# Rounded and remaining parts of w_out side by side: weight loads of the outputs step by two elements

## The reference

```python
qn = q / (np.linalg.norm(q, axis=1, keepdims=True) + 1e-06)
kn = k / (np.linalg.norm(k, axis=1, keepdims=True) + 1e-06)
s = kn.transpose(0, 2, 1) @ qn / tau          # B x 256 x 256
a = softmax(s, axis=-1)                        # written out in the reference
x = (v @ a).reshape(12032, 256)
h = x @ w_in                                   # 256 -> 2048
g = h * (1.0 / (1.0 + np.exp(-h)))
out = g @ w_out                                # 2048 -> 256
```

## Time and profile before

| | |
|---|---|
| median of 3 runs | 1107.22 us |
| profiled execution, its own time | 1106.86 us |
| its span (first to last instruction) | 1105.1 us |
| PE (matmuls) busy | 1096.5 us, 99% |
| PEld (weight loads) busy | 1080.7 us, 98% |
| DVE, ACT, POOL busy | 739.7, 646.0, 32.3 us |
| weight loads of the outputs | 3072, 188 ns each in the record |

### The profile page before, as it was taken

The page is one execution under the profiler, slowest core; times in us unless marked ns, Lnnn a source line. Parts: engine busy times, 40 slices in busy tenths (PEclk is TensorE's granted clock), DMA queues, the critical chain, the costliest instruction groups (busy, mean ns, idle before and its releaser), DMA issues.

```text
span 1105.1 us, 16789 instructions
## 1 busy us (share of the span) xinstructions
PE 1096.5 (99%) x6252; PEld 1080.7 (98%) x6252; DVE 739.7 (67%) x1188; ACT 646.0 (58%) x973; POOL 32.3 (3%) x24
## 2 busy tenths in 40 slices
PE   8999999999999999999999999999999999999998
PEld 7888999999999999999999999999999999999998
DVE  5776796666666665666687786666666666666654
ACT  5786765555555555555565655555564655555544
POOL 2440000000000000000000000000000000000000
PEclk9999999999999999999999999999999999999999
DMA  9990001010101000010100010010101000010000
GB/s 344 391 367 1 1 14 43 1 56 1 35 23 28 28 26 29 0 56 0 46 10 28 28 30 29 1 58 1 57 1 28 28 28 28 0 56 1 28 0 28
DMA packets 30019, 54.12 MB, mean 49 GB/s; under 512 B 2832, under 2 KB 21264, under 8 KB 29968
## 3 DMA queue, kind: packets, MB, share of 16 engines
q1 hardware_dynamic: 29968, 53.49, 13.7%
HBM read 41.16 MB, written 12.32 MB: 48 GB/s over the span
## 4 chain that ended last, share of the span: by engine, by line
PE 93%; DMA 3%; ACT 2%; DVE 1%; issue 1%; SPq 1%; ACTq 0%; DVEq 0%
PE ps_o L393 16%; PE ps_o L392 16%; PE ps_o L391 16%; PE ps_h L357 14%; PE ps_h L355 14%; PE ps_h L356 14%; DMA qk<-k_dram 3%; ACT ps_h L475 1%; PE ps_o L318 1%; DVE square_sum L646 0%; SPq L216 0%; PE ps_h L347 0%; PE ps_o L348 0%; PE ps_h L349 0%; PE ps_o L349 0%
## 5 line engine op out<-in xcount | busy, mean ns | idle before, releaser
L357 PE MATMUL ps_h<-b_hi,a_lo_rest 128*128 128x376 f32 x672 | 224.1, 333 | 0.0
L355 PE MATMUL ps_h<-b_hi,a_hi_rest 128*128 128x376 f32 x672 | 224.1, 333 | 0.0
L356 PE MATMUL ps_h<-b_lo,a_hi_rest 128*128 128x376 f32 x672 | 223.4, 332 | 0.0
L758 DVE TENSOR_TENSOR h_b<-ps_h,u 128x376 f32<-128x376 f32 x128 | 70.4, 550 | 163.8 <-PE ps_h L357 163.8
L739 DVE TENSOR_TENSOR u<-ps_h,u 128x376 f32<-128x376 f32 x128 | 70.3, 549 | 151.2 <-ACT u L547 137.0
L393 PE MATMUL ps_o<-g_hi_b,wo_lo 128*128 128x376 f32 x512 | 171.5, 335 | 0.0
L392 PE MATMUL ps_o<-g_lo_b,wo_hi 128*128 128x376 f32 x512 | 171.3, 335 | 0.0
L391 PE MATMUL ps_o<-g_hi_a,wo_hi 128*128 128x376 f32 x512 | 170.9, 334 | 0.0
L393 PE MATMUL ps_o<-g_hi_a,wo_lo 128*128 128x376 f32 x512 | 170.9, 334 | 0.0
L391 PE MATMUL ps_o<-g_hi_b,wo_hi 128*128 128x376 f32 x512 | 170.6, 333 | 0.0
L392 PE MATMUL ps_o<-g_lo_a,wo_hi 128*128 128x376 f32 x512 | 170.5, 333 | 0.0
(11 more groups left out here) (107 smaller groups left out, 1746.1 us busy)
## 6 DMA issues: line engine op xcount, KB each, us to landing
v_raw<-v_t_dram SPq DMA_DIRECT2D x64, 188.0 KB, 2.8
out_t_dram<-out_sb SPq DMA_DIRECT2D x32, 376.0 KB, 2.8
qk<-q_dram SPq DMA_DIRECT2D x25, 384.0 KB, 11.0
qk<-k_dram SPq DMA_DIRECT2D x25, 384.0 KB, 11.0
wp_raw<-w_out_dram SPq DMA_DIRECT2D x4, 512.0 KB, 11.7
wp_raw<-w_in_dram SPq DMA_DIRECT2D x4, 512.0 KB, 13.9
wp_raw<-q_dram SPq DMA_DIRECT2D x5, 384.0 KB, 10.9
wp_raw<-k_dram SPq DMA_DIRECT2D x5, 384.0 KB, 10.8
```

Of the source, the lines that this page charges most:

```text
L355: nc.tensor.matmul(ps_h[:, bank, 0:TOK], w_hi, x_hi, start=start, stop=False, skip_group_check=True)
L356: nc.tensor.matmul(ps_h[:, bank, 0:TOK], w_hi, x_lo, start=False, stop=False, skip_group_check=True)
L357: return nc.tensor.matmul(ps_h[:, bank, 0:TOK], w_lo, x_hi, start=False, stop=stop, skip_group_check=True)
L758: nc.vector.tensor_tensor(h_b[:, 0, :], ps_h[:, BANK_P5, 0:TOK], u[:], ALU.add).then_inc(c12_made, 1)
```

## The change

The two tensors `wo_hi` and `wo_lo`, each with its elements next to each other, become one tensor of the same total size in which each rounded element is followed by its remaining part. The two names are now views of it that step by two elements of 4 bytes. Everything that uses the names is the same text, and every engine issues the same instructions in the same order. What differs is the step in them: the 3072 weight loads of the outputs read 128 elements at a step of two, ScalarE's four roundings write 1024 elements at a step of two, and GpSimd's four subtractions read `wo_hi` and write `wo_lo` at a step of two.

```diff
         probs_lo = sb("probs_lo", [P, CK, C], F32R)
-        wo_hi = sb("wo_hi", [P, FK, C], F32R)
-        wo_lo = sb("wo_lo", [P, FK, C], F32R)
+
+        wo = sb("wo", [P, FK, C, 2], F32R)
+        wo_hi, wo_lo = (wo[:, :, :, i] for i in range(2))
```

## The result

| | before | after |
|---|---|---|
| median (8 runs each) | 1107.24 us | 1110.49 us |
| span of the profiled execution | 1105.1 us | 1108.7 us |
| ratio, 95% interval | | 1.0031 (1.0023 to 1.0040) |
| matmuls counted in 500 to 700 us | 1168 | 1164 |

The change made the kernel slower by 0.3%, outside the 0.2% within which I called it the same, though inside the range that I gave. The page of the changed kernel has the same picture of the third stage as before, only longer: full clock, and six lines with 90% of the chain. The shares of the first stage on the chain differ (7% matmuls of L319, 1% a DMA; before 1% and 3%), but the first fold starts only 0.17 us later.

The account below looks back on a forecast made before the run. It took the distance between TensorE's matmuls in the third stage, times their number, as the bound. All terms were put at 0 us, so it forecast the earlier median, 1107.2 us, with a range of 1103 to 1121 us.

Parts of the forecast that it names:

- the cover of 171 ns: Third stage: distance between two matmuls, 171.4 ns, in which a weight load of 110 ns must be done to stay unseen.
- rival 1: Output weight loads: step makes each slower than a matmul; at twice the time +149 us, 1256 us, up to 1302; chance 0.15.
- the 15 ns: Matmul distance beyond the columns' time, 14.7 ns at 376 columns, 16.3 at 512; perhaps the hand-over between sets of weights.
- part 1: The 3072 output weight loads at a step of two: hidden behind the matmul before, cost 0; upper bound +149 us.
- the sign of being wrong: Output lines: distance between matmuls moving by more than 0.7 ns either way, 2.2 us over 3072.
- rival 2: Output loads partly exposed: load 1.5 times as long, +26 us, or the 15 ns double, +46 us; chance 0.08.
- the near part of a rival: The share of rival 2, spread from 1109 to 1153 us, that the range up to 1121 us holds: chance 0.04.
- Rival 4: Loading stage: ScalarE's strided roundings partly not hidden, up to 4.2 us, giving 1109 to 1111 us; chance 0.03.
- parts 2 and 3: ScalarE's four roundings and GpSimd's four subtractions at a step of two: even at twice the time hidden by waits, 0 us.
- part 4: Whole kernel: same bytes in SBUF, no wait or buffer added, same order on every queue; cost 0.
- Rival 3: Outputs in the third stage: new layout removes up to 1.6 ns each, -4.9 us, 1102.3 us; chance 0.04.

Follow-up runs that it names:

- block: Against the kernel before: one tensor for both parts, per feature block 256 rounded then 256 remaining elements, so loads have no step; 1107.21 us, ratio 1.0004.
- fold2: Against the kernel before: rounded and remaining parts of the probabilities interleaved, so the fold's 96 loads step by two, w_out as before; 1107.64 us (one run).
- half2: Against the kernel before: two separate tensors kept, each interleaving the two halves of the output channels, so output loads step by two; 1110.55 us, ratio 1.0032.

## Why the prediction was wrong

**The bound** was read rightly: matmul distance times number is what counts, and the whole loss is in the distance.

**The load path** was read rightly: 110 ns without cover from one place in the trace, 111.7 measured; the cover of 171 ns; that a load longer than its cover sets the pace. The step of four is my rival 1 in full: I gave 1256 us, or 1302 with the 15 ns on top, and it came to 1300. That 1302 is so near is luck: the load takes 234 ns by itself at 128 as at 376 columns, and nothing comes on top of an uncovered load (111.7 ns at a step of one, not 125).

**The step that failed** is part 1: "What hides it is the matmul before, and it hides anything up to 1.4 times". A stepped load is 1.06 times as long (118.4 against 111.7 ns), far inside the cover, and still the distance grew by 0.94 ns, past the 0.7 ns that I had named as the sign of being wrong; 0.94 x 3072 = 2.9 us, most of the loss, stand in a term that I had put at 0. I took the cover as a threshold under which nothing is paid. The runs show that a covered load is paid for in part, and not in proportion to its length: 56 ns less of load takes off 1.3 ns, if half the elements take half of the 111.7 ns (an estimate; their record fell by 54); 7 ns more of load adds 0.9 at 376 columns, 1.3 at 256, 4 at 512. My rival 2 had the right kind of cause (part of a load is exposed) and the wrong sizes, 26 or 46 us where 3.3 came out; its first form needed a load 1.5 times as long, and its second, that the 15 ns are a piece of the load, is refuted for all but 1.3 ns by the run with 64 elements. Its spread began at 1109 us, so 1110.49 us lies in the range that I gave by the near part of a rival (chance 0.04 of 0.08) and not by the forecast. Rival 4 had such a number too, 1109 to 1111 us, but for another place.

**The writes** (parts 2 and 3) cost 4 x 0.11 us and 4 x 0.04 us and were hidden, as forecast; rival 4 is at most the 0.17 us by which the first fold is later, and block, without a step, starts it 0.11 us later too. The rest (part 4) held: block shows that placement costs nothing. Rival 3 (faster) didn't occur: the 12 outputs of the earlier trace rows with 172.5 ns were one stretch, and over the whole stage it is 171.71 against 171.25 ns.

**What stays open** is why a covered load costs anything. The two paces of one and the same fold suggest, but do not show, that loads and matmuls fall into a common rhythm and that a few nanoseconds of load shift it; the runs show the patterns, not their cause. That reads of weights collide with reads of the moving operand was not tried apart.

## What to carry to other kernels

A weight load with a step of two elements of 4 bytes is nearly free here (6% longer), one with a step of four takes twice the time and, beside 376 columns, sets the pace (+17.5% here). A covered operation is not free to the last nanosecond where 5760 of them stand in a row: 1 ns each is 0.3% for 3072. So keep weights next to each other, or at least two of them in 16 bytes (a step of three was not run). And where the loss must be told from no change, read the distance between starts over the whole stage from the trace, and not only the total: the mean for the outputs was 171.71 ns in three kernels without a step (before, block, fold2) and 172.65 in two with it (after, half2).

## What I had not expected of the hardware

- Loads of 128 elements of 4 bytes follow each other at 111.7, 118.4 and 234.1 ns for a step of one, two and four elements. The Trainium skill, "Advanced Engine Details and Errata", section SBUF Cachelines, has this shape: two hits in a line of 16 bytes hide the memory's delay, one does not. By it the step of two is free; the measurement says 6% on the load.
- The loads with a step of four take the same time at the lower granted clock: 235 ns at 0.50, where products went from 171 to 313 ns.
- ScalarE's writes of 1024 elements at these steps take 1.04, 1.15 and 2.07 us, GpSimd's subtraction 2.36, 2.40 and 2.92 us.
- Forty matmuls of 512 columns in a row, the same instructions at the same granted clock, are 228.9 ns apart in one trace and 233.3 ns in another, of a kernel that differs only elsewhere.
